# Loads without pacing waits at the start of a fused RWKV and mixture-of-experts kernel, u's load on the SP queue, and one DVE multiply a step earlier

## Chip, cores and metric

The kernel runs on one core of a Trainium2 chip. A core has five engines that run their own instruction streams and meet at semaphores: TensorE (PE), VectorE (DVE), ScalarE (ACT), GpSimd (POOL) and SyncE (SP). The metric is the device time in microseconds (us) of one execution; lower is better. Loads from memory are started by an instruction on an engine's queue (here mostly SP's) and carried out by 16 DMA engines; a semaphore reports when they have landed.

## What is computed

Three parts, each feeding the next. First an RWKV attention over 2 batches, 8 heads, 768 steps and head size 48; then an MLP with a squared ReLU over 1536 tokens (384 to 2048 to 384); then a top-1 mixture of 8 experts (384 to 1024 to 384).

```python
def _attn_ref(r, k, v, w, u):
    state = np.zeros((B, H, D, D))
    for t in range(S):
        kt, vt, rt, wt = (k[:, :, t], v[:, :, t], r[:, :, t], w[:, :, t])
        cur = np.einsum('bhd,bhe->bhde', u[None] * kt, vt)
        y[:, :, t] = np.einsum('bhd,bhde->bhe', rt, state + cur)
        state = wt[:, :, :, None] * state + np.einsum('bhd,bhe->bhde', kt, vt)

def _moe_ref(x, w_in, w_out):
    r = np.maximum(x @ w_in, 0.0)
    return (r * r) @ w_out

def _moe2_ref(x, w_gate, w1, w2, capacity):
    # the largest gate picks the expert, places are given in order up to capacity 384
    h = np.maximum(np.einsum('ecd,edf->ecf', disp, w1), 0.0)
    y = np.einsum('ecf,efd->ecd', h, w2)
    # out[i] = gate_w[i] * y[expert, place]
```

## The kernel before

The 1536 tokens are cut into 12 tiles of 128 steps, which go in pairs: group i (0 to 5) holds tiles (i, 0) and (i, 1), written (i, t). Attention works on the group ahead of the one that the MLP works on. Each engine has its own list of instructions written out in Python loops over groups i and 16 slots s; the lists are fixed, so an engine never overtakes a waiting instruction of its own. The tables `FIRST` and `LATER` say in which slot which step of attention stands.

**Attention of one group.** `KS` holds r, k and w of a tile: `ld_kr` reports the load of r and k (512 KB), `ld_wd` that of the decays w (256 KB). `mixed_weighted(i, t)` (DVE, L1201) multiplies part of it by `U`, `mixed_copied(i, t)` (ACT, L973 on KS) copies the other part. Then `first_level(i, t)` (PE, L612, 32 matmuls) computes the products inside single steps; `first_select` (DVE, L1231) puts them into the matrix `AD`, with the constant `eye`, which POOL builds at the very start (`made` reaches 2 at L516). `update` (DVE, L1217) scales `KS` in place by decays. Five more levels follow, each a `level` (PE, L628, 32 matmuls a tile), a `select` (DVE, L1242) and an `update` (DVE, L1217); the running products of the decays come from POOL in the first group (`first_totals`, L526). After the levels PE transposes the keys (L592), multiplies by `VV` (L647, L659) and by the state (L682), and the rows of x are split for the MLP into a high part `XH` (ACT, L973) and a low part `XL` (DVE, L1275).

**PE's order in the first group** is `first_level(0, 0)`, `first_level(0, 1)`, `level(0, 0, 1)`, `level(0, 1, 1)` and so on: the two tiles take turns.

**Weights.** A chunk is 128 x 1536 numbers (768 KB) of w_in (even chunks) or w_out (odd chunks), loaded into one of four `stage` buffers. ACT copies it into `W` as the high part (`L973 W<-stage`, 1.5 us) and DVE subtracts to get the low part (`split_low`, L1184, 1.75 us). In the first group ACT takes chunks 0, 1, 2, 3 in slots 0, 1, 6, 8 and DVE splits 0, 1, 2 in slots 5, 6, 7. `unread` (PE, L695) is a run of 9 and then 5 matmuls whose results nothing reads.

**SP's list at the start** issues the loads in the order that the diff below shows, with waits on DVE's progress (`upd[t]` counts the updates of tile t) and ACT's (`kn_ready`). A wait on `xl_ready[1]` stands before the second group's v, w_gate and chunk 4 (L403, L406), before and after the change alike. `U` is loaded from ACT's queue (L1098).

Of the kernel before, what the change touches and what calls it, by code (L numbers as in the profile page):

```python
# [5 lines left out]
def rwkv_moe_kernel(nc, cap, dims, krw, v, u, w_in, w_out, w_gate, w1, w2, gate_rows, out):  # L6
# [6 lines left out]
    DM, FF = w_in.shape  # L13
    N = B * S
    NE, _, FE = w1.shape
    HP = H // 2
    DP = 64
# [41 lines left out]
    with ctx:  # L59
        ctx.enter_context(nc.allow_non_contiguous_dma(reason="heads' rows of 192 bytes, u's columns"))  # L60

        def sb(name, shape, dt=F32, on=ctx):
            return on.enter_context(nc.sbuf_tensor(name, shape, dt))

        def sem(name):
            return ctx.enter_context(nc.semaphore(name))
# [52 lines left out]
        U = sb("U", [P, HP], on=p1)  # L119
# [62 lines left out]
        def mlp_chunk(n):  # L182

            if n % 2 == 0:
                cols = slice(n // 2 * CF, (n // 2 + 1) * CF)
                return w_in.rearrange("(k p) f -> p k f", p=P)[:, :, cols], [x[:, :, cols] for x in win], KM
            tiles = slice(n // 2 * CR, (n // 2 + 1) * CR)
            return w_out.rearrange("(f p) d -> p f d", p=P)[:, tiles, :], [x[:, tiles, :] for x in wout], CR
# [10 lines left out]
        def staged(c, parts):  # L199
            return stage[c][:, :].rearrange("p (a b) -> p a b", a=parts)  # L200
# [11 lines left out]
        ld_u, ld_gate = sem("ld_u"), sem("ld_gate")  # L212
# [8 lines left out]
        upd = [sem(f"upd{n}") for n in range(2)]  # L221
# [5 lines left out]
        kn_ready = [sem(f"kn_ready{n}") for n in range(2)]  # L227
# [36 lines left out]
        def need(eng, s, n):  # L264

            if not (isinstance(n, int) and n <= 0):
                eng.wait_ge(s, n)
# [101 lines left out]
        def _(sp):  # L369
            def load_tile(i, t):  # L370
                need(sp, xt_done[t], i - 1)
                need(sp, end_ready, 2 * (i - 2) + t + 1)
                for lo, hi, s in ((0, 2 * XW, ld_kr), (2 * XW, 3 * XW, ld_wd)):
                    sp.dma_start(KRW[t][i % 2][:, lo:hi], krw[2 * i + t, :, lo:hi]).then_inc(s[t][i % 2], 16)

            def load_v(i, t):
                need(sp, mid_read, 2 * (i - 2) + t + 1)
                sp.dma_start(VV[t][i % 2][:, :, :, :], v[2 * i + t]).then_inc(ld_v[t][i % 2], 16)


            def load_first(n):
                sp.dma_start(staged(n, mlp_chunk(n)[2]), mlp_chunk(n)[0]).then_inc(ld_w[n], 16)

            load_tile(0, 0)
            load_tile(0, 1)
            load_first(0)
            sp.wait_ge(upd[1], 1)
            load_first(1)
            sp.wait_ge(upd[0], 2)
            for t in range(2):  # L390
                load_v(0, t)
            sp.wait_ge(upd[0], 3)
            load_first(2)
            sp.wait_ge(upd[0], 4)
            load_tile(1, 0)
            sp.wait_ge(upd[0], 5)
            load_first(3)
            sp.wait_ge(kn_ready[0], 1)
            load_tile(1, 1)
            sp.wait_ge(xl_ready[1], 1)  # L400
            for t in range(2):
                load_v(1, t)
# [20 lines left out]
            def load_part(n):  # L423
                if n < CH * NE:
                    src, _, parts = expert_chunk(n // CH, n % CH)
                    sp.wait_ge(wl_ready, NW0 if n < RAW else NW0 + n - RAW + 1)
                    sp.dma_start(unsplit(n, parts), src).then_inc(ld_raw[n % RAW], 16)
# [44 lines left out]
            for e in range(NE):  # L472
                n = CH * (e + 1) + RAW
# [497 lines left out]
        def _(act):  # L971
# [48 lines left out]
            def body(i, attn, mlp, gate):  # L1020
                for s in range(NF):
# [38 lines left out]
                    if n is not None:  # L1060
                        _, parts, rows = mlp_chunk(n)
                        act.wait_ge(ld_w[n % CH], 16 * (n // CH + 1))
                        copy(parts[0], staged(n % CH, rows)).then_inc(wh_ready, 1)
# [26 lines left out]
            def split_high_expert(e, c):  # L1090
                if e >= NE:
                    return
                _, parts, rows = expert_chunk(e, c)
                n = CH * e + c
                act.wait_ge(ld_raw[n % RAW], 16 * (n // RAW + 1))
                copy(parts[0], unsplit(n, rows)).then_inc(wh_ready, 1)

            nc.scalar.dma_start(U[:, :], u).then_inc(ld_u, 16)  # L1098
            for t in range(2):
                mixed_copied(0, t)  # L1100
            pipeline(act, body)
# [77 lines left out]
        def _(dve):  # L1179
# [15 lines left out]
            def mixed_weighted(i, t):  # L1195

                dve.wait_ge(ld_kr[t][i % 2], 16 * (i // 2 + 1))
                need(dve, inc_done[t], i)
                out = every_second(UT[t][i % 2][:, 0:1], (2 - i % 2) * WIDTH + 1)
                x = every_second(KRW[t][i % 2][:, 0:1], XW + 1)  # L1200
                tt(out.rearrange("p r (q n) -> p r q n", q=HP), x.rearrange("p r (q n) -> p r q n", q=HP),  # L1201
                   U[:, :].rearrange("p (r q n) -> p r q n", r=1, n=1).to_broadcast([P, 2, HP, C]),
                   ALU.mult).then_inc(mixed_u[t], 1)

            def update(i, t, l):
                L = 1 << l
                if l == 0:
                    dve.wait_ge(ld_wd[t][i % 2], 16 * (i // 2 + 1))
                    dve.wait_ge(mixed_raw[t], i + 1)
                    dve.wait_ge(mixed_u[t], i + 1)  # L1210
                else:
                    dve.wait_ge(att[t], NSTEP * i + l + 1)
                    dve.wait_ge(upd[t], NL * i + l)
                    dve.wait_ge(tot[t], NL * i + l)
                x = halves(i, t, l)
                td = left_right(totals(i, t, l))
                tt(x, x, td.to_broadcast([P, 2, XW // (2 * L), L]), ALU.mult).then_inc(upd[t], 1)  # L1217

            def next_totals(i, t, l):

                if i > 0:
                    td = left_right(totals(i, t, l))
                    tt(totals(i, t, l + 1), td[:, 0, :, 0], td[:, 1, :, 0], ALU.mult).then_inc(tot[t], 1)

            def first_select(i, t):

                dve.wait_ge(att[t], NSTEP * i + 1)
                if i == 0:
                    dve.wait_ge(made, 2)
                    dve.wait_ge(cleared, 2)  # L1230
                nc.vector.copy_predicated(  # L1231
                    AD[t][:, :, :],
                    eye[:, :].bitcast(U32).rearrange("p (x n) -> p x n", x=1).to_broadcast([P, H, C]),
                    pair[t][:, :, :].rearrange("p a (q c) -> p (a q) c", q=HP)[:, :, 0:C]).then_inc(sel[t], 1)

            def select(i, t, l):
                L = 1 << l
                dve.wait_ge(att[t], NSTEP * i + l + 1)
                dve.wait_ge(sel[t], NMASK * i + l)
                got = pair[t][:, :, :].rearrange("p a (q c) -> p (a q) c", q=HP)[:, :, 0:C // 2]  # L1240
                m = mask[:, l, :].bitcast(U32).rearrange("p (o g j) -> p o g j", o=1, j=L)
                nc.vector.copy_predicated(  # L1242
                    AD[t][:, :, :].rearrange("p x (g two j) -> p x g two j", two=2, j=L)[:, :, :, 1, :],
                    m.to_broadcast([P, H, C // 2 // L, L]),
                    got.rearrange("p x (g j) -> p x g j", j=L)).then_inc(sel[t], 1)
# [151 lines left out]
            def split_low_expert(e, c):  # L1397
                if e >= NE:
                    return
                _, parts, rows = expert_chunk(e, c)  # L1400
                dve.wait_ge(wh_ready, NW0 + CH * e + c + 1)
                split_low(unsplit(CH * e + c, rows), parts)

            def step(n, t, k):
                if (n, t, k) == (0, 1, 0):
                    mixed_weighted(0, 1)
                if k == 0:
                    update(n, t, k)
                    first_select(n, t)
                else:  # L1410
                    if k < NMASK:
                        select(n, t, k)
                    update(n, t, k)
                next_totals(n, t, k)

            def body(i, attn, mlp, gate):
                for s in range(NF):
# [14 lines left out]
                    if k is not None and k < NL:  # L1432
                        step(n, 0, k)
                    elif k == NL + 1:
                        scale_start(n, 0)
# [6 lines left out]
                    if k is not None and k < NL:  # L1442
                        step(n, 1, k)
# [131 lines left out]
```

## Time and profile before

| what | value |
| --- | --- |
| runs | 450.08, 453.37, 453.95 us; median 453.37 |
| profiled execution, its own time | 450.08 us |
| span of its instructions | 448.1 us |
| PE busy | 427.2 us, 95% of the span |
| DVE, ACT, POOL busy | 68%, 58%, 13% |
| granted PE clock | 0.996 over the span |

The span runs from the first to the last instruction; the execution's own time is 2.0 us longer. A busy share says how much of the span the engine was at work, not that it was at its peak.

### The profile page before, as it was taken

To read this page: it belongs to the slowest core of one execution; us is meant where nothing else is said; L and a number is where in the kernel's file an instruction comes from. 1 tells how busy PE (TensorE), PEld (TensorE's weight loads), DVE (VectorE), ACT (ScalarE), POOL (GpSimd) and SP (SyncE) were. 2 spreads that over 40 slices of the span, in tenths; PEclk is the share of its full clock that TensorE was granted. 3 is DMA by queue.
4 is the path that set the end of the run, shared out by engine and by line. 5 is a ranking of instruction groups with operands and counts; after the bars stand their busy time and mean duration, and the time that the engine had idled before them with its cause. 6 is when DMAs were issued, how large, how long until landed. Compare 5 with 4: busy or idle time off the path is not lost.

```text
span 448.1 us, 14525 instructions
## 1 busy us (share of the span) xinstructions
PE 427.2 (95%) x5882; PEld 405.4 (90%) x5882; DVE 303.9 (68%) x763; ACT 257.7 (58%) x527; POOL 57.0 (13%) x77
## 2 busy tenths in 40 slices
PE   2899999999999999999999999999999899999994
PEld 2778999999999999999999999989997789999994
DVE  4996966766777767777778637558538877687510
ACT  3366766546644664466546665573648875686421
POOL 6400000000000200010001000301030333421201
PEclk9999999999999999999999999999999999999998
DMA  6847976850400131010001094522885998520001
GB/s 217 287 145 241 354 260 237 312 222 3 170 29 1 39 132 66 1 39 2 3 3 38 4 327 169 194 72 77 302 262 169 346 336 292 168 63 2 30 2 45
DMA packets 35642, 63.39 MB, mean 141 GB/s; under 512 B 3980, under 2 KB 21950, under 8 KB 35568
## 3 DMA queue, kind: packets, MB, share of 16 engines
q1 hardware_dynamic: 33120, 57.87, 38.0%
q0 software_dynamic: 2304, 4.47, 2.7%
q8 instruction: 54, 0.88, 0.8%
q14 instruction: 20, 0.16, 0.1%
q10 hardware_dynamic: 144, 0.00, 0.0%
HBM read 50.77 MB, written 14.19 MB: 145 GB/s over the span
## 4 chain that ended last, share of the span: by engine, by line
PE 87%; DVE 3%; issue 3%; ACT 2%; DMA 1%; POOL 1%; POOLq 0%; SPq 0%; DVEq 0%; ACTq 0%
PE bank L721 22%; PE bank L707 22%; PE bank L934 6%; PE pair L628 6%; PE bank L887 5%; PE pair L592 3%; PE pair L887 3%; PE pair L902 3%; PE bank L941 3%; PE bank L902 3%; PE pair L647 2%; PE pair L682 1%; DMA stage<-in_moe_w_in 1%; ACT W L973 1%; PE pair L934 1%
## 5 line engine op out<-in xcount | busy, mean ns | idle before, releaser
L707 PE MATMUL bank<-XH,W 128*128 128x256 f32 x576 | 118.7, 284 | 0.7 <-ACT RB L1077 0.7
L721 PE MATMUL bank<-W,GH 128*128 128x384 f32 x372 | 98.3, 345 | 0.0
L707 PEld LDWEIGHTS bank<-XH,W 128*128 128x128 f32 x576 | 94.9, 188 | 1.7 <-issue 0.9
L707 PE MATMUL bank<-XL,W 128*128 128x256 f32 x288 | 80.6, 280 | 0.0
L1280 DVE TENSOR_TENSOR GL<-GG,GH 128x256 fp32r<-128x256 f32 x96 | 40.4, 421 | 35.0 <-ACT GH L973 31.9
L1077 ACT ACTIVATE RB<-bank 128x256 f32<-128x256 f32 x96 | 36.6, 381 | 47.1 <-PE bank L707 46.0
L721 PEld LDWEIGHTS bank<-W,GH 128*128 128x128 f32 x372 | 61.7, 188 | 1.2
L721 PE MATMUL bank<-W,GL 128*128 128x384 f32 x186 | 62.6, 336 | 0.0
L973 ACT ACTIVATE GH<-GG 128x256 fp32r<-128x256 f32 x96 | 40.2, 418 | 34.1 <-PE bank L721 32.3
L707 PEld LDWEIGHTS bank<-XL,W 128*128 128x128 f32 x288 | 54.3, 189 | 0.0
L1217 DVE TENSOR_TENSOR KS<-KS 128x512 f32<-128x512 f32 x72 | 49.8, 693 | 6.1 <-PE pair L628 5.8
L1184 DVE TENSOR_TENSOR W<-raw,W 128x1536 fp32r<-128x1536 f32 x23 | 40.1, 1753 | 9.5 <-ACT W L973 9.5
L1083 ACT ACTIVATE GG<-RB 128x256 f32<-128x256 f32 x96 | 40.0, 417 | 2.1 <-DVE GL L1280 0.2
L1242 DVE COPY_PREDICATED AD<-mask,pair 128x256 f32<-128x256 uint32 x48 | 24.4, 508 | 24.6 <-PE pair L628 24.5
L934 PE MATMUL bank<-W,HH 128*128 128x384 f32 x192 | 38.9, 344 | 0.0
L628 PE MATMUL pair<-KS 48*62 48x32 f32 (+4 forms) x1920 | 34.0, 221 | 1.9 <-DVE KS L1217 1.3
L628 PEld LDWEIGHTS pair<-KS 48*62 48x62 f32 (+4 forms) x1920 | 29.9, 136 | 6.5 <-DVE KS L1217 2.4
L721 PEld LDWEIGHTS bank<-W,GL 128*128 128x128 f32 x186 | 34.9, 188 | 0.0
L563 POOL DMA_INDIRECT slots<-X,slot_u x8 | 8.3, 1040 | 199.1 <-DVE slot_u L1386 185.0
L973 ACT ACTIVATE W<-raw 128x1536 fp32r<-128x1536 f32 x23 | 33.5, 1479 | 0.0
L1184 DVE TENSOR_TENSOR W<-stage,W 128x1536 fp32r<-128x1536 f32 x17 | 29.7, 1754 | 5.5 <-ACT W L973 5.5
L934 PEld LDWEIGHTS bank<-W,HH 128*128 128x128 f32 x192 | 33.2, 188 | 0.0
(164 smaller groups left out, 711.5 us busy)
## 6 DMA issues: line engine op xcount, KB each, us to landing
raw<-in_moe_w SPq DMA_DIRECT2D x23, 768.0 KB, 7.6
stage<-in_moe_w SPq DMA_DIRECT2D x9, 768.0 KB, 7.8
KS<-in_krw SPq DMA_DIRECT2D x12, 512.0 KB, 5.9
slots<-X SPq DMA_DIRECT2D x8, 579.0 KB, 6.5
VV<-in_v SPq DMA_DIRECT2D x12, 288.0 KB, 6.2
KS<-in_krw SPq DMA_DIRECT2D x12, 256.0 KB, 6.1
stage<-in_moe_w_in SPq DMA_DIRECT2D x4, 768.0 KB, 6.6
stage<-in_moe_w_out SPq DMA_DIRECT2D x4, 768.0 KB, 6.7
```

What stands on the lines that cost most here:

```text
L628: last = nc.tensor.matmul(pair[t][to:to + n, a, q * P:q * P + C // 2], x[rows, XW + c:XW + c + n], right_of(x[rows, 0:XW], c, l), start=q ...
L707: last = nc.tensor.matmul(bank[4 + f % 2][:, 0:2 * P], win[wa][:, c, f * P:(f + 1) * P], xa[:, c, :], start=n == 0, stop=n == 3 * KM - 1)
L721: last = nc.tensor.matmul(bank[6 + m][:, 0:DM], ga[(NF * g + f) % G3][:, cols], wout[wa][:, f, :], start=f == 0 and n == 0, stop=f == NF - ...
L887: last = nc.tensor.matmul(bank[HB[f % 3]][:, 0:2 * P], w1s(e, wa)[:, c, f * P:(f + 1) * P], xa[:, c, 0:2 * P], start=n == 0, stop=n == 3 * ...
L902: last = nc.tensor.matmul(bank[SMALL[m][c]][:, 0:CF], xa[:, k_, m * P:(m + 1) * P], w1s(e, wa)[:, k_, c * CF:(c + 1) * CF], start=n == 0, ...
L934: nc.tensor.matmul(y, HH[:, f, cols], w2s(e, wa)[:, f, :], start=f == 0 and wa == 0, stop=False)
L973: return nc.scalar.activation(dst, src, ACT.Copy)
L1077: nc.scalar.activation(RB[:, :], bank[4 + f % 2][:, 0:2 * P], ACT.Relu).then_inc(relu_ready, 1)
L1083: nc.scalar.activation(GG[f % 2][:, :], RB[:, :], ACT.Square).then_inc(g_ready, 1)
L1184: return tt(parts[1], src, parts[0].bitcast(F32), ALU.subtract).then_inc(wl_ready, 1)
L1217: tt(x, x, td.to_broadcast([P, 2, XW // (2 * L), L]), ALU.mult).then_inc(upd[t], 1)
L1280: tt(GL[k][:, :], GG[f % 2][:, :], GH[k][:, :].bitcast(F32), ALU.subtract).then_inc(gl_ready, 1)
```

## The change

It touches only the first 30 us or so. U's load moves from ACT's queue to third place on SP's; the waits before chunk 1, the v loads and tile (1, 0) go; tile (1, 1) moves ahead of chunks 2 and 3, behind the wait `upd[0] >= 3`; the waits `upd[1] >= 1`, `upd[0] >= 2`, `upd[0] >= 4` and `kn_ready[0] >= 1` are gone, and those on `upd[0] >= 3`, `upd[0] >= 5` and `xl_ready[1] >= 1` stay. On DVE, `mixed_weighted(0, 1)` stands ahead of `update(0, 0, 0)` and `first_select(0, 0)` instead of behind them.

```diff
+            load_tile(0, 0)
+            sp.dma_start(U[:, :], u).then_inc(ld_u, 16)
+            load_tile(0, 1)
+
             def load_first(n):
                 sp.dma_start(staged(n, mlp_chunk(n)[2]), mlp_chunk(n)[0]).then_inc(ld_w[n], 16)
 
-            load_tile(0, 0)
-            load_tile(0, 1)
-            load_first(0)
-            sp.wait_ge(upd[1], 1)
-            load_first(1)
-            sp.wait_ge(upd[0], 2)
+            for n in range(2):
+                load_first(n)
             for t in range(2):
                 load_v(0, t)
+            load_tile(1, 0)
             sp.wait_ge(upd[0], 3)
+            load_tile(1, 1)
             load_first(2)
-            sp.wait_ge(upd[0], 4)
-            load_tile(1, 0)
             sp.wait_ge(upd[0], 5)
             load_first(3)
-            sp.wait_ge(kn_ready[0], 1)
-            load_tile(1, 1)
             sp.wait_ge(xl_ready[1], 1)
             for t in range(2):
                 load_v(1, t)
...
-            nc.scalar.dma_start(U[:, :], u).then_inc(ld_u, 16)
             for t in range(2):
                 mixed_copied(0, t)
             pipeline(act, body)
...
             def step(n, t, k):
-                if (n, t, k) == (0, 1, 0):
+                if (n, t, k) == (0, 0, 0):
                     mixed_weighted(0, 1)
                 if k == 0:
                     update(n, t, k)
```

On DVE, the first instructions of the first group before the change are these (KS0 and KS1 are tiles (0, 0) and (0, 1), L1201 is `mixed_weighted`, L1217 `update`, L1231 `first_select`; the waits are the semaphores that the instruction needs):

```order
L1201 TENSOR_TENSOR KS0<-KS0,U 128x2x256 [waits ld_kr00,ld_u]
L1217 TENSOR_TENSOR KS0<-KS0 128x2x256 [waits mixed_u0,mixed_raw0,ld_wd00]
L1231 COPY_PREDICATED AD0<-eye,pair0 128x512 [waits cleared,made,att0]
L1201 TENSOR_TENSOR KS1<-KS1,U 128x2x256 [waits ld_kr10]
L1217 TENSOR_TENSOR KS1<-KS1 128x2x256 [waits mixed_u1,mixed_raw1,ld_wd10]
L1231 COPY_PREDICATED AD1<-eye,pair1 128x512 [waits cleared,made,att1]
```

On DVE, the same place after the change, where all lines stand 3 lower (L1198 is `mixed_weighted`, L1214 `update`, L1228 `first_select`):

```order
L1198 TENSOR_TENSOR KS0<-KS0,U 128x2x256 [waits ld_kr00,ld_u]
L1198 TENSOR_TENSOR KS1<-KS1,U 128x2x256 [waits ld_kr10]
L1214 TENSOR_TENSOR KS0<-KS0 128x2x256 [waits mixed_u0,mixed_raw0,ld_wd00]
L1228 COPY_PREDICATED AD0<-eye,pair0 128x512 [waits cleared,made,att0]
L1214 TENSOR_TENSOR KS1<-KS1 128x2x256 [waits mixed_u1,mixed_raw1,ld_wd10]
L1228 COPY_PREDICATED AD1<-eye,pair1 128x512 [waits cleared,made,att1]
```

The multiply of tile (0, 1) stands two places earlier; both updates and both selects keep their order behind it.

On SP, the loads of the first group after the change (SP's queue is the one on which all of them are issued; stage0 to stage3 take chunks 0 to 3, VV is v):

```order
L374 DMA KS0<-in_krw 128x512
L382 DMA U<-in_u 128x4
L374 DMA KS1<-in_krw 128x1024
L374 DMA KS1<-in_krw 128x512
L386 DMA stage0<-in_moe_w_in 128x3x512
L386 DMA stage1<-in_moe_w_out 128x4x384
L378 DMA VV00<-in_v 128x576
L378 DMA VV10<-in_v 128x576
L374 DMA KS0<-in_krw 128x1024
L374 DMA KS0<-in_krw 128x512
L374 DMA KS1<-in_krw 128x1024 [waits upd0]
```

Before, stage1 waited for upd1, the first v for upd0, and both loads into KS0 and KS1 of the second group stood behind chunk 2; now ten loads stand between the start and SP's first wait.

## Rows read from the trace of the kernel before

**Rows 1.** The page: busy time and its share of the span, by engine.

```profile
PE 427.2 (95%) x5882; PEld 405.4 (90%) x5882; DVE 303.9 (68%) x763; ACT 257.7 (58%) x527; POOL 57.0 (13%) x77
```

**Rows 2.** Chain of waits, 7 to 12 us: start, length, what.

```profile
7.29 0.26 POOL eye L516
...
7.63 0.73 DVE AD L1231
8.36 0.58 DVE KS L1201
...
9.08 1.13 PE pair L612 x32
10.21 0.83 PE pair L628 x32
```

**Rows 3.** Timeline, 0 to 12 us: start, length, instruction, idle before it and its releaser.

```profile
4.73 0.67 ACT L973 ACTIVATE KS<-KS 128x512 f32<-128x512 f32 x1 [2.22 <-DMA KS<-in_krw]
4.93 0.73 DVE L1201 TENSOR_TENSOR KS<-KS,U 128x512 f32<-128x512 f32 x1 [2.93 <-DMA U<-in_u]
6.69 0.67 ACT L973 ACTIVATE KS<-KS 128x512 f32<-128x512 f32 x1 [1.28 <-DMA KS<-in_krw]
...
9.07 0.69 DVE L1217 TENSOR_TENSOR KS<-KS 128x512 f32<-128x512 f32 x1
...
10.27 0.74 DVE L1231 COPY_PREDICATED AD<-eye,pair 128x512 f32<-128x512 uint32 x1 [0.51 <-PE pair L612]
...
11.07 0.73 DVE L1242 COPY_PREDICATED AD<-mask,pair 128x256 f32<-128x256 uint32 x1
```

**Rows 4.** DMA queues, 0 to 10 us: packets, MB, share; then issues, median us to landing.

```profile
q10 hardware_dynamic: 144, 0.00, 0.8%
...
U<-in_u ACTq DMA_DIRECT2D x1, 2.0 KB, 4.1
```

**Rows 5.** Chain of waits, 20 to 33 us.

```profile
25.50 0.50 ACT IN L973
...
26.71 1.77 PE bank L695 x9
28.48 0.66 PE pair L682 x32
...
30.81 0.57 DVE XL L1275
```

**Rows 6.** The same chain, 31 to 40 us.

```profile
32.72 6.48 DMA stage<-in_moe_w_in
...
39.22 1.49 ACT W L973
```

**Rows 7.** Busy time by stretch: PE, PEld, DVE, ACT, POOL, PEclk, DMA share, GB/s.

```profile
5.00:6.00 1.00, 0.19 (x8) 0.22 (x12) 0.87 (x2) 0.41 (x1) 1.00 (x3) 1.00 1.03 414
9.00:10.00 1.00, 0.92 (x34) 0.95 (x38) 0.69 (x1) 0.65 (x1) 0.00 (x0) 1.00 0.00 0
18.00:20.00 2.00, 1.51 (x72) 1.24 (x76) 1.94 (x5) 0.46 (x2) 0.00 (x0) 1.00 0.94 289
```

**Rows 8.** Timeline, 18 to 28 us: SP's issue of chunk 3, ACT and DVE.

```profile
18.78 0.38 SPq L382 DMA_DIRECT2D stage<-in_moe_w_out  x1
...
21.22 5.18 DVE L1184 TENSOR_TENSOR W<-stage,W 128x1536 fp32r<-128x1536 f32 x3
...
23.13 1.48 ACT L973 ACTIVATE W<-stage 128x1536 fp32r<-128x1536 f32 x1
...
26.32 0.35 DVE L1269 TENSOR_TENSOR SD<-IN,KS 128x192 f32<-128x192 f32 x1
26.36 1.49 ACT L973 ACTIVATE W<-stage 128x1536 fp32r<-128x1536 f32 x1
```

**Rows 9.** Issue of chunk 3, 18.5 to 19 us: KB, us to landing.

```profile
stage<-in_moe_w_out SPq DMA_DIRECT2D x1, 768.0 KB, 7.6
```

**Rows 10.** DMA queues, 10 to 12 us: instruction blocks.

```profile
q8 instruction: 1, 0.02, 4.6%
```

## The prediction

> **What bounds the kernel now.** I read the page first: PE is busy for 95% of the span [rows 1], so over the whole run an edit that does not shorten PE's list cannot take much. The edit touches only the first 30 us, and there PE is not the bound, so the question is what the first group waits for. The chain of waits tells [rows 2]: POOL finishes the constant `eye` at 7.55 us (7.29 + 0.26), that releases DVE's `first_select` of tile 0 at 7.63, behind it stands `mixed_weighted` of tile 1, which ends at 8.94, then PE does 32 first-level matmuls of tile 1 (9.08, 1.13 us) and only then, since the two tiles take turns on PE, level 1 of tile 0 at 10.21. The reader is to see that tile 1's data were not what was late: ACT began its copy of them at 6.69, at once when they landed [rows 3]. The multiply of tile 1 stood in DVE's queue behind a select that waited for POOL. DVE paid again: before the select of tile 1 at 10.27 it sat idle 0.51 us for PE's first level [rows 3]. From 11.07 on DVE and PE pass levels to each other, up to the handover to the MLP at about 31 us [rows 3, 5].
>
> Behind that a second thing carries time: SP issues chunk 4 at 32.72, because it stands behind the wait on `xl_ready[1]`, it takes 6.48 us to land, and ACT copies it at 39.22 [rows 6]. The change leaves this wait and its place. `xl_ready[1]` comes from the XL step at 30.81 [rows 5], so whatever the first group gains or loses moves this load by as much, and then PE's full list: a shift of the first group should reach the end unchanged.
>
> **The DVE swap.** It adds no instruction; it exchanges places. The new times are built from landings. Tile 1's r and k landed by 6.69 in the trace [rows 3]. U's load now stands ahead of them in SP's queue. What it costs there no row shows. From below: its 144 packets took 0.8% of 16 engines over 10 us, 0.08 us [rows 4]. From above: the issue of one load on SP, about 0.38 us [rows 8]. The loads of tile 1 are limited by the transfer (414 GB/s with all engines at work, [rows 7]) and not by their issue, so I stand nearer to the lower end and take 0.2. The multiply of tile 1 then starts at 6.89. From there DVE has five steps in a row before it reaches the select of tile 1: that multiply (0.73), the update of tile 0 (0.69), its select (0.73), the update of tile 1 (0.69) [rows 2, 3]. 6.89 + 0.73 + 0.69 + 0.73 + 0.69 = 9.73, where the select of tile 1 starts; it started at 10.27. **Gain 0.54 us**, with U's bounds 0.36 to 0.66. The things it waits for are there: `eye` at 7.55, and tile 0's select starts at 8.31; PE's first level of tile 1 starts when the multiply ends at 7.62, or when tile 0's is through, and takes 1.13, so it ends at about 8.8. Level 1 of tile 0 on PE can start at about 9.05 instead of 10.21, so PE is the earlier of the two, and the DVE chain sets the gain.
>
> **U from SP's queue.** This makes the multiply of tile 0 later and nothing else. It started at 4.93, when U landed, 4.1 us after an issue at 0.80 [rows 3, 4]. Two loads now go ahead of it, at 0.38 to 0.42 us each, so the issue is at about 1.65 and the landing, at the same 4.1 us, at 5.75. The multiply ends at 6.48 and PE's first level of tile 0 at about 7.65, with the select of tile 0 at 8.31 still covered. The cover ends when U lands after 6.16 (6.89 less 0.73); from then each us of lateness costs a us. Taking the DMA issue off ACT saves nothing: ACT waited 2.22 us for the tile afterwards [rows 3].
>
> **Loads without waits.** Chunk 1, v and tile (1, 0) are now queued by about 6 us, behind all that the first level needs, and fill the time in which the DMA engines did nothing (9 to 10 us: 0 GB/s, [rows 7]). None was waited for on the chain after 7 us, so their earliness gains nothing: chunk 1's low part is split only at 21.22, in DVE's fixed order [rows 8]. Cost nothing, under one cover: chunk 2. It now stands behind tile (1, 1). Ahead of its end, after chunk 0, are chunk 1, two v loads, two tiles and chunk 2 itself: 4 x 0.786 + 0.59 = 3.74 MB. From 9.35 us on (ACT's first weight copy) that takes 9.3 us at 400 GB/s and 12.9 us at 289 GB/s, the rate of 18 to 20 us [rows 7], so it lands between 18.7 and 22.3. ACT wants it at 22.6 (23.13 less 0.54, [rows 8]). It fits, with 0.3 us to spare at the slow end. Chunk 3 took 7.6 us and landed at 26.4, when ACT took it [rows 8, 9]; it is issued as before, with tile (1, 1) moved from behind it to ahead of it, which is 0.786 MB or 2 to 2.7 us of queue, against the gaps in which the engines did nothing before. It should land at about 25.8 at the latest, when ACT is free for it. Behind ACT's copy of chunk 3 stands only a copy of tile 0's rows, and PE's 9 unread matmuls (1.77 us, [rows 5]) cover a part of its lateness.
>
> **The sum.** 450.08 (the profiled execution's own time, span 448.1 and 2.0 around it) - 0.54 + 0 + 0 = 449.5. This execution is the fastest of three; the others, 453.37 and 453.95, are 3.3 and 3.9 us above it, and no row explains that. Two of three runs lie at the upper place, so the median to expect is 453.37 - 0.54 = 452.8.
>
> **A rule weighed.** The instruction stream comes over the same 16 DMA engines: between 10 and 12 us one block took 4.6% of them [rows 10]. The Trainium skill, "DMA: Bandwidth & Descriptors", section "Queues, rings and completion order", says that an engine goes round its queue rows in turn, packet by packet. By that an instruction block does not stand behind the 3 MB that the change queues, only behind one packet, and the sum stays; if it stood behind them, the fourth rival below would be likely. No row of this trace has a block beside so deep a queue, so I keep the rival with a small chance.
>
> **The rivals.**
> 1. Forecast: the DVE chain starts from tile 1's landing, 449.5 on this execution's scale, 452.8 as a median. For it: the idle 0.51 us and the multiply parked behind POOL [rows 2, 3]. Chance 0.60.
> 2. U is late. If it lands at 6.7 (5.05 us after its issue instead of 4.1), the multiply of tile 0 ends at 7.43 and the four steps lead to 10.27 again: no gain, 450.1, or 453.4 as a median. For it: U is now behind 768 KB in one queue; against it: those are through by about 5.4 us (the next 512 KB landed at 6.69, at 414 GB/s). Chance 0.2. Here the change also may not do what it seems to: all of it lies under other waits.
> 3. Slower: chunk 2 lands late. Its limit is 22.6 for ACT, and the DVE split that follows ends in front of the state steps (26.32, four of 0.35 us and their waits, about 28.0) that PE needs at 28.48 [rows 5, 8]; that slack of 0.45 makes the limit 23.1. At 289 GB/s and with a tail of 2.5 us (chunk 3 shows that one 768 KB load can take 7.6 us, [rows 9]) it would land at 24.8, 1.7 us past that: 449.5 + 1.7 = 451.2, as a median 454.5. It turns the sign when it lands later than 23.6. Chance 0.13.
> 4. Slower: an instruction block is held up by the deep queue. One block's own engine time is 4.6% of 16 engines over 2 us, 1.5 us [rows 10]; once more of it on the chain gives 449.5 + 1.5 = 451.0, 454.3 as a median. Chance 0.05.
> The last 0.02 is for what I don't see.
>
> **How the numbers follow.** A measurement of this kernel tells about 1% (4.5 us) from no change. All cases lie within 1.7 us of before; only the scatter of the runs (0.9% between fastest and slowest) could carry a median over that bound, more easily downwards, where the fast place at 450 is with a gain: same 0.93, faster 0.05, slower 0.02. The range holds the forecast at both places of the runs, from 450.08 less 0.66 (449.4, and 0.1 for scatter below it) to 454.5 for the third rival; rivals 2 and 4 lie inside. Its width is almost all the scatter of the runs; the effect alone is -0.66 to +1.2.
>
> **What the profile after would show.** The multiply of tile 1 at 6.8 to 7.1, right behind that of tile 0 (5.4 to 5.8); tile 0's select at 8.2 to 8.5 with no wait for `eye`; tile 1's select at 9.6 to 9.9 with no idle time; every later step of the first group 0.4 to 0.7 us earlier, chunk 4's issue at 32.2, and no wait of ACT for chunk 2 or 3. Rival 2 would show U as the releaser of the first multiply later than 6.2; rival 3 ACT idle for `stage` at about 23; rival 4 engines idle on "issue" between 8 and 18 us. The prediction fails if the shift at 32 us is not there at the end, or if the runs fall into places other than the two shown.

## The result and the profile after

The changed kernel is slower: median 455.71 us of 15 runs (454.30 to 456.47), against 451.79 us of 15 runs before (450.08 to 455.14); ratio 1.0077, 95% interval 1.0058 to 1.0096. The ratio goes by the means, by which the loss is 3.5 us; the medians lie 3.9 us apart. The profiled execution took 453.21 us (span 451.2) and the one of before 450.08 (span 448.1).

The page says that no engine has more to do: PE is busy 427.7 us against 427.2 [rows 1]. The time went into waiting. The waits of PE in the first 35 us, the changed kernel (waiter, releaser, total, times, longest):

```profile
PE pair L610 <- DVE KS L1198: 7.8, 2, 6.2
PE pair L626 <- issue: 2.9, 2, 2.2
```

"issue" means that PE waited for nothing that the profile shows. The chain of waits of the changed kernel, 2 to 43 us, in the places that answer to [rows 2, 5, 6]:

```profile
2.18 5.91 DMA KS<-in_krw
8.09 0.02 issue
8.11 0.70 DVE KS L1198
8.81 0.14 issue
8.95 1.13 PE pair L610 x32
...
10.19 1.11 PE pair L626 x32
...
13.84 1.95 PE pair L626 x60
15.79 0.72 issue
16.52 0.43 PE pair L626 x4
...
20.06 0.64 PE pair L626 x26
20.70 2.20 issue
22.89 0.36 PE pair L626 x6
...
34.47 0.57 DVE XL L1272
...
36.40 5.82 DMA stage<-in_moe_w_in
```

Three things are to be seen. The load of tile (0, 1) is now on the chain and lands at 8.09. In spite of it level 1 of tile 0 starts at 10.19, as before [rows 2], so the swap gave back the landing and no more. And PE stops twice in the middle of a level, once after 28 of the 32 matmuls of level 3 of tile 0 (0.72 us; the 60 are 32 of level 2 and these 28) and once after 26 of 32 of level 5 (2.20 us). No semaphore stands there. The XL step comes at 34.47 instead of 30.81 [rows 5], 3.66 us later; chunk 4 is issued at 36.40 instead of 32.72 and lands 5.82 instead of 6.48 us later [rows 6], so 3.0 us are left, and the spans differ by 3.1.

What PE lacks at these points is code. The DMA view of the changed kernel, 14 to 16 us (queue: packets, MB, share of 16 engines):

```profile
q1 hardware_dynamic: 148, 0.32, 44.6%
q8 instruction: 1, 0.02, 3.3%
```

The same view over 11 to 14 us has no q8 packet, though q1 keeps the engines full:

```profile
q1 hardware_dynamic: 552, 1.23, 104.2%
```

One q8 packet holds 16 KB; that these packets are PE's instructions is read from the counts that follow and from the run `pad` below. Narrowing this view's window gives the start of each such block to 0.05 us: before 10.95, 15.85 and 22.70; after 14.22, 20.61 and 25.91. Counting PE's pairs (a weight load and its matmul) from the start, the first stop is before pair 221, the second before pair 347. Between them lie 126 pairs and 4 single semaphore instructions, 256 instructions. By the same count the block before ends behind pair 94.

### The profile page after: what moved, and what is told of

Read it like the earlier page. It is cut to its first block, busy times and chain, and to the rows that moved or that the text cites. A ratio compares the mean times of both kernels' runs of the same rounds, so it can differ in the third digit from the quotient of the medians.

```text
span 451.2 us, 14525 instructions
## 1 busy us (share of the span) xinstructions
PE 427.7 (95%) x5882; PEld 405.8 (90%) x5882; DVE 303.3 (67%) x763; ACT 257.5 (57%) x527; POOL 57.1 (13%) x77
## 4 chain that ended last, share of the span: by engine, by line
PE 87%; issue 3%; DVE 3%; ACT 3%; DMA 3%; SPq 1%; POOLq 0%; DVEq 0%; ACTq 0%
PE bank L719 22%; PE bank L705 22%; PE pair L626 6%; PE bank L932 6%; PE bank L885 5%; PE pair L590 4%; PE pair L885 3%; PE pair L900 3%; PE bank L939 3%; PE bank L900 3%; PE pair L645 2%; PE pair L680 1%; DMA KS<-in_krw 1%; DMA stage<-in_moe_w_in 1%; PE pair L657 1%
## 5 line engine op out<-in xcount | busy, mean ns | idle before, releaser
L1214 DVE TENSOR_TENSOR KS<-KS 128x512 f32<-128x512 f32 x72 | 49.6, 690 | 8.1 <-PE pair L626 8.0
```

## The experiments

Sixteen runs were made, three of them repeats (`before_again`, `after_again`, `swap_again`); `pad` and `gaps_pad` stand below the table. Ratios are against the kernel before, run beside them on the same chip; a row without one was run once (after_again 455.43, swap_again 453.69, gaps_no_swap 453.53 us), and each profile is one execution. The columns are times in us from the span's start: tile (0, 1) taken by ACT (the start of its second copy), the start of pair 95 and of PE's first block, and likewise for pair 221 and the second block. "Stop" is PE's idle time that ends on issue before pairs 221 and 347, and before pair 472 or 473.

| run | tile 1 | pair 95, block | stop 221 | pair 221, block | stop 347 | stop 472 | ratio (95%) |
| --- | --- | --- | --- | --- | --- | --- | --- |
| before | 6.69 | 10.72, 10.95 | 0 | 15.25, 15.85 | 0 | 0.21 | |
| before_again | 6.52 | 11.02, 11.86 | 0 | 15.55, 15.89 | 0 | 1.14 | |
| after | 8.11 | 10.97, 14.22 | 0.72 | 16.52, 20.61 | 2.20 | 0 | 1.0077 (1.0058 to 1.0096) |
| after_again | 7.13 | 10.05, 14.78 | 2.36 | 17.23, 20.05 | 1.11 | 0.29 | |
| swap_only | 7.05 | 9.98, 13.64 | 1.28 | 16.09, 18.43 | 0.55 | 0.40 | 1.0037 (1.0008 to 1.0065) |
| swap_again | 7.08 | 10.44, 14.18 | 1.01 | 16.59, 18.56 | 0.29 | 0.46 | |
| u_only | 7.51 | 11.01, 11.88 | 0 | 15.55, 18.74 | 1.29 | 0 | 1.0016 (0.9992 to 1.0040) |
| u_and_swap | 7.36 | 10.63, 14.64 | 1.29 | 17.05, 19.00 | 0 | 0.23 | 1.0058 (1.0028 to 1.0089) |
| loads_only | 7.15 | 11.10, 13.99 | 0.58 | 16.52, 20.74 | 2.48 | 0 | 1.0041 (1.0017 to 1.0064) |
| deeper | 7.59 | 11.00, 11.21 | 0 | 15.54, 17.47 | 0.28 | 0 | 0.9993 (0.9963 to 1.0023) |
| hold_one | 8.32 | 11.18, 13.52 | 0.16 | 16.16, 21.41 | 3.59 | 0 | 1.0099 (1.0062 to 1.0136) |
| tiles_late | 7.81 | 11.01, 13.76 | 0.18 | 16.01, 18.72 | 0.84 | 0.29 | 1.0009 (0.9976 to 1.0042) |
| two_gaps | 7.24 | 10.52, 12.88 | 0 | 15.37, 16.53 | 0 | 1.20 | 1.0032 (1.0003 to 1.0061) |
| gaps_no_swap | 7.10 | 10.71, 11.26 | 0 | 15.24, 16.22 | 0 | 0.86 | |
| slim | 7.47 | 10.69, 10.89 | 0 | 15.22, 17.89 | 1.02 | 0 | 0.9995 (0.9964 to 1.0025) |
| slim_swap | 7.18 | 10.44, 15.76 | 2.67 | 18.25, 20.22 | 0.28 | 0.29 | 1.0061 (1.0035 to 1.0088) |

The table fits one sum. Wherever PE stopped for one of its first two blocks, it went on 2.2 to 2.6 us after that block's start (after: 14.22 to 16.52, 20.61 to 22.89; loads_only: 20.74 to 23.17; hold_one: 21.41 to 23.91). PE's own work from pair 95 to pair 221 takes 4.5 us and from pair 221 to pair 347 3.9 us (before: 10.72 to 15.25, 15.25 to 19.17). So the first block may start 2.1 us after pair 95 and the second 1.5 us after pair 221; what is later becomes a stop. In the changed kernel the second is 4.1 us late: 4.1 + 2.3 - 3.9 = 2.5. From start to start the two matmuls lie 2.4 us apart; the stop of 2.20 is counted from the end of the last one, so each stop in the table is about 0.25 us shorter than the time lost.

A late block seems to make the next one late as well. Where PE had stopped at pair 221, the second block never started less than 1.95 us after that pair (swap_again, u_and_swap and slim_swap: 1.95 to 1.97), against 0.3 to 1.2 us in before, before_again, gaps_no_swap and two_gaps.

**The parts, one by one.** `swap_only` is the DVE hunk of the diff alone, `u_only` moves the load of U, `u_and_swap` is both, and `loads_only` has

```diff
             load_first(0)
-            sp.wait_ge(upd[1], 1)
             load_first(1)
-            sp.wait_ge(upd[0], 2)
             for t in range(2):
                 load_v(0, t)
+            load_tile(1, 0)
             sp.wait_ge(upd[0], 3)
+            load_tile(1, 1)
             load_first(2)
-            sp.wait_ge(upd[0], 4)
-            load_tile(1, 0)
             sp.wait_ge(upd[0], 5)
             load_first(3)
-            sp.wait_ge(kn_ready[0], 1)
-            load_tile(1, 1)
```

Expected of swap_only: 

> The kernel before with the DVE swap alone: the multiply of tile (0, 1) stands ahead of the update and select of tile (0, 0); U stays on ACT's queue, all waits of SP stay. Both theories (instruction blocks held up by a deep queue; the tile's load slowed by U's small pieces or by later loads) say the swap is harmless: tile (0, 1) lands at 6.7, its select starts at about 9.6 instead of 10.27, chunk 4 is issued at about 32.1 instead of 32.7, and the time is 0.5 us below before. If the swap itself were to blame, chunk 4 would be issued later than 33.

Measured: slower, 1.0037. The multiply of tile 1 ran at 7.05, pair 95 came 0.7 us sooner than in the kernel before, and then PE stopped, on the rows of PE's timeline in swap_only:

```profile
16.09 1.15 PE L628 MATMUL pair<-KS 48*56 48x32 f32 x36 [1.28 <-issue]
20.82 0.78 PE L628 MATMUL pair<-KS 48*32 48x32 f32 x38 [0.55 <-issue]
```

The first step of my sum was there and more than given back; chunk 4 was issued at 34.13, past the 33 that was named as the sign against the swap. Neither theory had expected that.

Expected of u_only: 

> The kernel before with U's load in third place on SP's queue and nothing else changed. Theory A (U's 128 pieces of 16 bytes hold up the loads behind them in the same queue): ACT's copy of tile (0, 1) starts at about 7.9 to 8.1 as in the changed kernel, against 6.69 before; since the multiply stands behind the first select, which ended at 8.36, little of it reaches the chain: +0 to +0.5 us. Theory B (the later loads slow the tile): it lands at 6.8, +0.1 us at most. Both: no idle time of PE on issue over 0.5 us.

Measured: ACT took tile 1 at 7.51, between the two; the time is not told apart from before, though this profile has a stop of 1.29, which both theories had excluded.

Expected of loads_only: 

> The kernel before with the load list of the changed kernel (no waits before chunk 1, v and tile (1, 0); tile (1, 1) ahead of chunks 2 and 3), but U on ACT's queue and no swap. Theory of the instruction blocks: PE is idle on issue for 0.7 and 2.2 us at about 16 and 21 us, its blocks start at about 14 and 20.5 instead of 10.8 and 15.8, chunk 4 is issued at about 36, and the time is 3 to 3.5 us above before. Rival (the late tile landing under U's pieces started the delay): chunk 4 is issued below 34 and the time is within 1.3 us of before. Whether the first tile's load lands at 6.7 or at 8 tells if later loads in the queue slow it.

Measured: both stops as expected (0.58 and 2.48; blocks at 13.99 and 20.74), chunk 4 issued at 36.52, the time 1.0041, which is 1.9 us and less than the 3 to 3.5 expected. Tile 1 landed at 7.15: the later loads in the queue did not slow it.

Expected of u_and_swap: 

> The kernel before with U on SP's queue and the DVE swap, all of SP's waits kept. Theory of the instruction blocks: their starts stay at about 10.8 and 15.8, PE has no idle time on issue over 0.5 us, and the time lies between -0.5 us (if the tile lands at 6.9) and +0.3 us (if it lands at 8.1). Rival (U and the swap carry the loss): chunk 4 is issued at 35 or later and the time is 3 us above before.

Measured: 1.0058 with all of SP's waits kept. That fell outside what I allowed to the theory of the blocks with the queue as their only cause: the first block started at 14.64 and PE stopped for 1.29 us.

**Is it code?** The changed kernel with 40 instructions more at the head of PE's list:

```diff
+            place(40)
             pe.wait_ge(made, 1)
             pipeline(pe, body)
```

Expected of pad: 

> The changed kernel with 40 semaphore instructions more at the head of PE's list, nothing else. Theory of the instruction blocks (16 KB, 256 instructions each, PE stops when it reaches the end of a block whose successor is not there): the two idle times on issue move 40 instructions, or 20 pairs of weight load and matmul, forward: from before the 221st and 347th pair to before the 201st and 327th; the first grows by up to 0.6 us since PE gets there sooner. Rival (something that PE's work waits for, a semaphore or data): the idle times stay at the 221st and 347th pair.

Measured, on PE's timeline of pad:

```profile
16.71 1.53 PE L626 MATMUL pair<-KS 48*56 48x32 f32 x56 [1.85 <-issue]
22.28 1.06 PE L626 MATMUL pair<-KS 48*32 48x32 f32 x58 [1.31 <-issue]
```

The changed kernel's stops have 36 and 38 matmuls behind them in the same groups, here there are 56 and 58: both stops moved by exactly 20 pairs, or 40 instructions, forward. What PE waits for is tied to a count of instructions, not to data or a semaphore. The first was longer, 1.85 instead of 0.72, but the unpadded kernel had 2.36 there when profiled again, so that says nothing. (455.32 us, one run.)

**Is it chance?** Expected of before_again: 

> The kernel before, unchanged, profiled a second time on another execution. Its first profile was of one of its fastest executions (450.08 against a median of 452.5 in the later rounds). Theory of the instruction blocks: PE's block starts lie a varying time after PE asks for them, so a typical execution of 452 to 453 us has an idle time on issue of 1 to 2 us at the 221st or 347th pair of weight load and matmul, which the first profile lacks. Rival (the scatter is elsewhere): the first 30 us are as in the first profile and the difference lies later.

Measured: 452.38 us, with one stop, in PE's timeline of before_again, where the first profile had 0.21 us:

```profile
25.82 0.92 PE L659 MATMUL pair<-VV,KS 64*64 64x48 f32 x49 [1.14 <-issue]
```

It is at pair 472, a block later than I had expected, and chunk 4 was issued at 33.56 instead of 32.72. The kernel before, too, waits for code in some executions.

Expected of swap_again: 

> The swap alone, profiled again. If the late first block (13.64) is a property of the swap, it starts at 13 to 14.5 again and PE stops 1 to 2 us at the 221st pair; if it was chance, it starts within 1 us of the 95th pair (about 10.5 to 11).

Measured: first block at 14.18, a stop of 1.01. The late block came again with the swap.

Expected of after_again: 

> The changed kernel, profiled again. The theory of the blocks expects the two idle times at the 221st and 347th pair again, together 3 us or more, and the landing of tile (0, 1) at 7.7 or later.

Measured: stops of 2.36 and 1.11, together 3.5, as expected; but tile 1 was taken at 7.13. Its late landing (8.11) was mostly chance and the loss is there without it.

**The queue's depth.** `deeper` issues chunk 3 right behind chunk 1 in the kernel before:

```diff
             sp.wait_ge(upd[1], 1)
             load_first(1)
+            load_first(3)
             sp.wait_ge(upd[0], 2)
...
             sp.wait_ge(upd[0], 5)
-            load_first(3)
```

Expected of deeper: 

> The kernel before with chunk 3 issued right behind chunk 1 instead of after the fifth update: 768 KB more in the queue when PE asks for its first block, the same loads in all. Theory of the instruction blocks: the first block starts about 4 us after the 95th pair or later, PE stops 1.5 to 3 us at the 221st pair, time 1 to 2 us above before's median. Rival (depth does not matter): no idle time at the 221st pair beyond what before shows, the time within 0.2% of before.

Measured: my theory missed. The first block started at 11.21, 0.2 us after pair 95, and the time is that of before. These loads are issued at about 10 us, and the block's packet is then ahead of their data. What seems to count is what is queued before PE asks, not behind it.

`hold_one` puts one wait back into the changed kernel:

```diff
+            load_first(0)
+            sp.wait_ge(upd[0], 2)
+            load_first(1)
-            for n in range(2):
-                load_first(n)
             for t in range(2):
                 load_v(0, t)
```

Expected of hold_one: 

> The changed kernel with one wait put back: chunk 1 and all loads behind it wait for the second update of tile (0, 0), so that the DMA engines are empty from 9.3 to about 13 us, when PE asks for its first block; the rest of the list stays as dense as in the changed kernel. Theory of the instruction blocks: the first block starts by 13 us and PE does not stop at the 221st pair; the second is asked for at about 15.5 with 3.7 MB in the queue and starts 3 us late or more, so PE stops 1.5 us or more at the 347th pair; time 0.5 to 1.5 us below the changed kernel's, still above before. Rival (the loss is the early landing of tile 1 or the swap): both idle times stay as in the changed kernel.

Measured: the stops moved as expected, on PE's timeline of hold_one:

```profile
16.16 1.14 PE L627 MATMUL pair<-KS 48*56 48x32 f32 x36 [0.16 <-issue]
23.91 0.78 PE L627 MATMUL pair<-KS 48*32 48x32 f32 x38 [3.59 <-issue]
```

With the DMA engines empty the first block started 2.3 us after pair 95, and the first stop nearly went (0.16, against 0.72 and 2.36 in the two profiles of the changed kernel). The backlog behind it made the second block 5.2 us late, and that stop took 3.59 us (2.20 and 1.11 there). The time did not fall as expected: 1.0099, whose interval overlaps that of the changed kernel. I had mis-sized the second stop.

`tiles_late` is the changed kernel with both tiles of the second group behind `kn_ready`:

```diff
-            load_tile(1, 0)
             sp.wait_ge(upd[0], 3)
-            load_tile(1, 1)
             load_first(2)
             sp.wait_ge(upd[0], 5)
             load_first(3)
+            sp.wait_ge(kn_ready[0], 1)
+            load_tile(1, 0)
+            load_tile(1, 1)
```

Expected of tiles_late: 

> The changed kernel with tiles (1, 0) and (1, 1) loaded only after kn_ready of tile 0 instead of early: 1.5 MB less in the queue between 8 and 20 us. Theory of the instruction blocks: the first block is still late (chunk 0, chunk 1 and v in the queue: idle at the 221st pair 0 to 1.5 us), the second starts within 2 us of the 221st pair, idle time at the 347th pair below 0.8 us against 2.4; time 1.5 to 2.5 us below the changed kernel's. Rival: what is queued does not matter, the idle times stay at 1.0 and 2.4.

Measured: time 1.0009 (0.9976 to 1.0042), more gained than expected. 1.5 MB less in the queue takes back most of the loss, with the swap and U's load still as in the changed kernel. At which block is not told by one profile: the two stops are 0.18 and 0.84 here, 0.72 and 2.20 or 2.36 and 1.11 in the changed kernel, whose second block came 4.1 and 2.8 us after pair 221, here 2.7.

**Where in the queue a block starts.** The DMA view from 0 us on counts what q1 has moved. Both tiles of the first group and chunk 0 are 2.36 MB, a further chunk or tile is 0.79 MB, the two v loads are 0.59 MB. In tiles_late, from 0 to the start of the first block (0 to 13.75 us) and of the second (0 to 18.7 us):

```profile
q1 hardware_dynamic: 1936, 3.74, 78.9%
```

```profile
q1 hardware_dynamic: 2326, 4.52, 70.8%
```

3.74 MB is all up to the v loads, 4.52 all up to chunk 2, and these are just the loads that SP had issued: each block started when the queue ahead of it was done. Counted in the same way, the blocks of the changed kernel started at 4.29 and 6.05 MB of 4.52 and 6.09 issued, those of loads_only at 4.30 and 6.10, the first of swap_only at 3.16, behind chunk 1. In the kernel before they started at 2.37 and 3.74 MB, ahead of chunk 1 and of chunk 2, and deeper's first at 2.37, ahead of both chunks. Two second blocks started in the middle of a load (hold_one 4.99, slim 4.80). This fits that a load delays a block if it is issued before PE's request and not if it is issued after, though no record tells when PE asks.

**Two attempts at a better order.** `two_gaps` has the swap, and chunk 1 behind `upd[0] >= 2`, v, chunk 2 and tile (1, 0) behind `upd[0] >= 4`, chunk 3 behind 5, tile (1, 1) behind `kn_ready`.

Expected of two_gaps: 

> The DVE swap, U on ACT's queue, and loads placed so that the DMA engines are empty when PE asks for its first two blocks: chunk 1 waits for the second update of tile (0, 0), then v, chunk 2 and tile (1, 0) for the fourth, chunk 3 for the fifth, tile (1, 1) for kn_ready. Theory of the instruction blocks: the first block starts within 0.5 us of the 95th pair, the second within 1 us of the 221st, no idle time on issue at the 221st or 347th pair, chunk 4 issued at about 32.2, time 2 to 3 us below the median of before. Rival (the swap itself is at fault): the time is at or above before's, as with the swap alone (+0.37%).

Measured: no stop at pairs 221 and 347, but 1.0032, and the first block came 2.4 us after pair 95, not within 0.5. PE stopped 1.20 us at pair 472 and was slow afterwards. PE has nine large matmuls on W next. In PE's timeline of before_again they take 1.83 us:

```profile
27.49 1.83 PE L695 MATMUL bank<-W 128*128 128x384 f32 x9
```

In two_gaps the same nine take

```profile
28.63 3.25 PE L693 MATMUL bank<-W 128*128 128x384 f32 x9
```

The stop alone did not bring that about: before_again stopped 1.14 us at the same pair and then took 1.83 us. And PE was slow in two_gaps before its stop, in the 15 matmuls just ahead of it, here in two_gaps

```profile
24.46 0.64 PE L657 MATMUL pair<-VV,KS 64*64 64x48 f32 x15
```

and in before_again

```profile
24.28 0.40 PE L659 MATMUL pair<-VV,KS 64*64 64x48 f32 x15
```

The windows view prints a granted clock of 1.00 for this stretch in both, but the trace's clock record begins only at 33.3 us in two_gaps and at 23.9 us in before_again (24.5 in before, 25.1 in gaps_no_swap). Where it begins, the matmuls turn fast: in tiles_late, whose record begins at 30.8, the nine on W start 0.32 us apart up to 30.6 and 0.17 us apart from 30.9 on. So before the record it is the durations that show the lower of the two levels, 1.2 GHz. Until 33 us two_gaps worked at that level: from pair 472 to the first XL step it took 7.8 us, before_again 5.2 us. The record begins late in after_again (33.3), slim_swap (33.5) and tiles_late (30.8) too, each with a stop of only 0.29 at pair 472. That the stops hold the clock back is possible and not shown. This late rise, more than the stop, ate the gain of the profiled execution.

`slim` is the kernel before with chunk 3 behind chunk 1, both tiles of the second group behind `kn_ready`, `slim_swap` the same with the swap.

Expected of slim: 

> The kernel before with chunk 3 behind chunk 1 and both tiles of the second group behind kn_ready, no swap, U on ACT's queue: nothing is in the queue from about 20 to 23 us. Theory of the instruction blocks: the first as in the run with chunk 3 early (start 0.2 us after the 95th pair), the second 1 to 2.5 us after the 221st pair (idle 0 to 0.8 us), the third within 1 us of the 347th pair, so no idle time at the 472nd pair, where before shows 0.2 and 1.4; time 0.5 to 1.5 us below before. Rival (before's pacing is already as good as it gets, or other scatter dominates): within 0.2% of before.

Measured: 0.9995, no gain: the first block 0.2 us after pair 95, the second 2.7 us after pair 221 (stop 1.02), which undid the stop at pair 472 that it took away.

Expected of slim_swap: 

> The same with the DVE swap. If the swap is harmless by itself it gains the 0.5 us of the first step: 1 to 2 us below before. The three runs with the swap so far had the first block 2.4 to 4.0 us after the 95th pair, so the other outcome is an idle time of 1 to 1.6 us at the 221st pair and a time at or above that of the run without the swap.

Measured: the other outcome, a stop of 2.67 and 1.0061. Two kernels that differ in the swap alone: 0.9995 against 1.0061.

**Why the swap makes the first block late.** Expected of gaps_no_swap (two_gaps without the swap): 

> The load list of the run with two gaps, without the DVE swap. The DMA engines are empty when PE asks for its first block, as there, and only the DVE order differs. If the swap makes PE ask later or makes the block wait, the block starts 0.2 to 0.9 us after the 95th pair here, against 2.4 with the swap; if the queue alone decides, it is 2.4 here too.

Measured: 0.55 us after pair 95 against 2.36 with the swap, the DMA engines empty in both (no packet at all from 10 to 12 us in two_gaps). So the swap delays the block by 1.8 us without any queue; hold_one, with the swap and empty engines too, has 2.3 us. With loads in the queue it is more: 3.7, 3.7 and 4.0 us in swap_only, swap_again and u_and_swap, behind chunk 1, and 5.3 in slim_swap, behind chunks 1 and 3.

Expected of gaps_pad (two_gaps with `place(70)` at the head of PE's list): 

> The run with two gaps and the swap, with 70 semaphore instructions more at the head of PE's list, so that the end of its first block falls before the 60th pair, ahead of the wait that stands before the 65th, instead of behind the 94th. If PE asks when its sequencer passes the end of a block, the first block starts 1.5 us or more earlier than 12.88. If it is tied to the wait before the 97th pair, it stays within 0.5 us of 12.88. The next ends of blocks move to the 185th, 311th and 437th pair.

Measured: inconclusive as it was meant. Each added instruction costs PE 0.15 us from start to start, so that its first matmul came at 11.72 instead of 6 us, in PE's timeline of gaps_pad:

```profile
11.72 1.98 PE L610 MATMUL pair<-KS 48*64 48x64 f32 x64 [11.72 <-issue]
```

The block started at 13.59, neither earlier by 1.5 us nor within 0.5 us of 12.88. It is 0.3 us after pair 60 began and ahead of pairs 65 (13.79) and 97 (15.00). This fits a request at the end of a block (behind pair 59 here) and speaks against one tied to the wait before pair 97. It also shows a prompt block with the swap, where PE no longer waited between its first pairs. Later stops came behind pairs 311 and 436; 311 and 437 were foretold. (464.84 us, one run.)

## Why the prediction was wrong

It forecast 452.8 us within 449.3 to 454.5, unchanged with a gain of 0.54 us; measured were 455.7 and a loss of 3.5 us. The two terms of the sum that failed are the loads, put at 0, and the swap, put at -0.54.

**"Loads without waits ... Cost nothing, under one cover: chunk 2."** This step failed. I asked which load was waited for and looked only at data. The waits that the change removes kept the queue short when PE asked for code; without them, and with nothing else changed (loads_only), the blocks started 2.9 and 4.2 us after pairs 95 and 221 instead of 0.2 to 0.8 and 0.3 to 0.6. That run puts the price at 0.41% (0.17 to 0.64), 1.9 us. (SP issues eleven loads before its first wait, not the ten of the list ahead of the prediction, and the last at 6.81 us.) The cover that I did name held: neither after nor loads_only has ACT waiting for chunk 2 or 3.

**The rule weighed, and rival 4.** I had the right mechanism as a rival, "an instruction block is held up by the deep queue", with 0.05 and 1.5 us. Its chance was set low since the Trainium skill, "DMA: Bandwidth & Descriptors", section "Queues, rings and completion order", says that an engine goes round its queue rows packet by packet. The runs do not bear out what I made of it, that a block stands behind one packet only: with 1.23 MB moved on q1 between 11 and 14 us none started, and tiles_late's blocks started when all 3.74 and 4.52 MB issued before them had moved. No record tells when PE asks, so this goes by the counts and not by a measured wait. It also mattered twice, not once, and the price of one late block is not its 1.5 us of transfer but its delay less the 2.1 or 1.5 us that PE can cover.

**"Gain 0.54 us" of the swap.** The DVE steps came in the order worked out and without idle time, and 0.4 us faster (8.11 to the select of tile 1 at 10.53, 2.42 us; the sum had 2.84 for what it calls five steps and lists as four). With the load at 7.05, in swap_only, pair 95 came 0.7 us sooner. But the swap alone costs 0.37% (0.08 to 0.65), and its two profiles show a late first block and stops of 1.28 and 1.01 at pair 221. In the five profiles with the swap and SP's waits it starts 2.4 us (two_gaps) to 5.3 us (slim_swap) after pair 95, in the six with such waits and without the swap (before, before_again, u_only, deeper, slim, gaps_no_swap) 0.2 to 0.9 us after it. Nothing in the trace of before showed that code could be short at pair 221: there it had 2 us to spare. But a sign of late code stood in that trace, at pair 472, 2.3 us after the block that started at 22.70, and I did not read it. In PE's timeline of before:

```profile
24.98 0.92 PE L659 MATMUL pair<-VV,KS 64*64 64x48 f32 x49 [0.21 <-issue]
```

**"The multiply of tile 1 then starts at 6.89."** Two errors. The base of 6.69 was one execution's: with U on ACT's queue eleven profiles have 6.52 to 7.59, median 7.15. And U's load costs more than the 0.2 taken: the seven profiles with U on SP's queue have 7.13 to 8.32, median 7.72, so about 0.6 us instead of 0.08 to 0.38, though the two groups overlap. In time this part is not resolved (1.0016, 0.9992 to 1.0040). Rival 2 did not come true: U was not late, its multiply ran at 5.37. What ate the swap's gain in the profile of the changed kernel was the landing of tile (0, 1), and in after_again, with 7.13, not even that.

**Carry to the end.** Right, but for the size: 3.66 us at the XL step, 3.1 at the end, since chunk 4 landed 0.66 us faster.

**The range.** It was drawn around two places of three runs. Fifteen runs have no such places; before spreads over 450 to 455 us, and the profiled execution was one of the fastest, with blocks that came early. The repeat, 452.38 us, has a stop of 1.14. So the profile from which I summed lacked the very wait that decides.

**What stays open.** The ratios of the parts, 0.37% and 0.41%, add up to about the 0.77% of the whole (U's load, 0.16%, is not told apart from nothing), but with intervals this wide the sum proves no more than that no third part is needed. Why the swap delays the first block with empty DMA engines is not settled. Without it PE is still at the first level of tile 1 when it may go on past pair 65; with it PE stands idle for 0.5 us before pair 65 in two_gaps and swap_again, but for only 0.2 us in swap_only, whose block was 3.7 us late. That the request is sent later for this reason is an argument, not shown; no record tells when PE asks.

## What to carry to other kernels

Loads that nobody waits for are not free: they stand in the same DMA engines as the code, and a block can start only when they are done (tiles_late: at 3.74 and 4.52 MB), and an engine with many small instructions (here 256 in about 4 us) needs a block every few us and stops when it is late. Before taking away waits that only pace loads, look for the instruction packets in the DMA view and for idle time on "issue" in the middle of a group. And profile the kernel before more than once when its runs scatter by more than the effect, since its fastest execution may lack the wait that counts.

## What was not expected of the hardware

- PE's code comes in 16 KB packets of 256 instructions, here 126 pairs; the packet that starts near pair 95 holds what PE needs from pair 221 on. After a stop PE went on 2.2 to 2.6 us after a block's start, though its packet took 0.9 to 1.1 us.
- Most block packets started about when the loads issued ahead of them had moved (tiles_late: 3.74 and 4.52 MB). In the kernel before, chunk 1 was issued at 9.79 and the block, at 10.95, still went ahead of it.
- The stop moves with the number of instructions: 40 more at the head, 20 pairs earlier, to the pair.
- A semaphore-only instruction on PE costs 0.15 us.
- The landing of one and the same early load varied from 6.5 to 7.6 us over eleven profiles with U on ACT's queue.
- The clock record of a trace can begin late (23.9 to 35.5 us here), and the views print 1.00 before it. Nine matmuls took 3.25 us at the lower level and 1.83 at the full one.
